# Gate logits of the fifth token group on VectorE within the last group of a fused attention and mixture-of-experts kernel, with a new order of the routing steps

## The chip, the cores and the metric

The kernel runs on one core of a Trainium2 chip. The metric is the device time of one execution in microseconds (us), taken as the median of several runs; lower is better.

## The reference

Three blocks follow one another. A linear attention with a decaying state gives a 3072 x 512 activation. A gated feed-forward block maps it through `(x @ w_a) * (x @ w_b) @ w_out` with 1536 hidden columns. A mixture of eight experts then sends each token to one expert.

```python
x = _moe_ref(x, ...)                        # (x @ w_a) * (x @ w_b) @ w_out
logits = x @ w_gate                         # 3072 x 8, the expert gates
e_idx = np.argmax(logits, axis=1)
probs = np.exp(logits - logits.max(-1, keepdims=True))
probs /= probs.sum(-1, keepdims=True) + 1e-09
gate_w = probs[np.arange(N), e_idx]
eom = 1.0 / (1.0 + np.exp(-(x @ w_output_gate)))   # 3072 x 8, the output gates
for e in range(E):
    mask = e_idx == e
    ye = np.maximum(x[mask] @ w1[e], 0.0) @ w2[e]
    out[mask] = gate_w[mask, None] * eom[mask, e, None] * ye
```

## The kernel before, in words

The 3072 tokens are cut into six groups of 512 (g = 0 to 5), each of four tiles of 128 tokens. In the feed-forward stage every group runs twelve steps, f = 0 to 11. In step f TensorE makes the two products of 128 hidden columns (`pe_up`, 24 matmuls of 512 columns, the b half first and then the a half) and after it the output product of the step before (`down`, 12 matmuls). VectorE multiplies the halves into `g_sb`, ScalarE rounds that to `g_hi`, VectorE makes the rest `g_lo`, and `down(f)` waits for `g_lo(f)`. Step 0 has no `down` of its own group ahead of it, but the last `down` of the group before has been issued already, so step 1 follows step 0 after 24 matmuls. After step 11 ScalarE evicts the group's output to `y_sb` and SyncE stores it to `x_rows` in the chip's memory.

The gates of group g - 1 are worked out during group g, from `y_sb`. The work has five parts: the 16 logits of each token, `dve_choose` (the best expert of each token), `dve_seen` (a running count of tokens by expert, which signals `seen_done`), the rank of each token within its expert (two small matmuls in `pe_rank`, which waits for `seen_done`, and `dve_rank`), and the scale (`dve_own_gate` picks the output gate of the chosen expert, `dve_scale` writes `t_scale`).

The logits of groups 0 to 3 are row products on VectorE (`dve_dots`): 64 instructions of 128 x 512, one for each of 16 gate columns and each of four tiles. Each reads a gate row that SyncE has broadcast to all partitions; there are four row buffers, so row e is loaded once the products of row e - 4 are done. `DOTS_AT` says how many of the 64 products stand in each step. The logits of group 4, which are worked out in the last group, g = 5, are made on TensorE: in steps 0 to 3 it transposes one tile each (`pe_yT`), in step 4 it multiplies by the gates (`pe_partial`) and in step 5 it adds the partial sums (`pe_logits`), and VectorE copies each result out of bank 3.

The first expert tiles (slots) are gathered ahead of time, from the tokens of groups 0 to 4 alone. `dve_off_hot` and `dve_first_hot` make one-hot tables from the ranks, `pe_first_slots` sorts with 20 small matmuls, and `dve_first_slots` writes the indices and signals `first_ready`. GpSimd's gathers 0 and 1 wait for `first_ready`, for the stored rows of group 4 (`x_out`) and for its stored scales (`scale_out`, which follows `t_scale` by one SyncE transfer). TensorE transposes the tile of gather 0 (`x_T`) after the `pe_up` of step 11 and ahead of `down(10)`. Every queue is in program order; nothing is scheduled at run time.

Of the kernel before, what the change touches and what calls it, by code (L numbers as in the profile page):

```python
# [5 lines left out]
F32R = mybir.dt.float32r  # L6
# [6 lines left out]
P = 128  # L13
# [15 lines left out]
GT = 512  # L29
# [63 lines left out]
def build(nc, steps_in, weights_in, gates_in, w1_in, w2_in, const_in, xT_dram, x_dram, out):  # L93
# [114 lines left out]
    gate_row = [place(f"gate_row{n}", (P, DM)) for n in range(GATE_SLOTS)]  # L208
    products_at = at[0]
    products = place("products", (P, DM))  # L210
    yT_sb = place("yT_sb", (P, KD, GT), where=yT_sb_at)
    part_sb = place("part_sb", (P, GT), where=products_at)
    gates_T = place("gates_T", (P, P), where=products_at)
    assert yT_sb_at + KD * GT * 4 <= products_at

    at[0] = products_at
    id_first = place("id_first", (P, TILES - TG))
    eq_first = place("eq_first", (P, TILES - TG, FIRST))
    hot_first = place("hot_first", (P, TILES - TG, FIRST), F32R)
    inv_first = place("inv_first", (P, FIRST))  # L220
    pad = place("pad", (P, 1))


    at[0] = common
# [44 lines left out]
    tl_i, tl_e, tl_run = (place(f"tl_{n}", (P, COLS + 1)) for n in range(3))  # L269
    tl_cmp, tl_cmp2 = (place(f"tl8_{n}", (P, COLS + 1, NE)) for n in range(2))  # L270
    off_hot = place("off_hot", (P, TILES, P), F32R)
    assert at[0] <= w2_lo_at + 2 * KE * DM * 4

    bank = [nc.alloc_psum_tensor(f"bank{i}", [P, 512], F32).ap() for i in range(8)]
# [363 lines left out]
    seen_done, rank_done, rank_read = sem("seen_done"), sem("rank_done"), sem("rank_read")  # L638


    AT_PART, AT_LOGITS = TG, TG + 1
    AT_CHOOSE, AT_GATE, AT_SCALE, AT_RANK = 6, 7, 8, 9
    DOT_CHOOSE, DOT_SEEN, DOT_RANK, DOT_SCALE = 6, 7, 10, 11
    LINKS = 15 + TG
    AT_FIRST = 10
    AT_W1_HI = {5: (0, 1), 6: (2, 3)}
    AT_W1_LO = {AT_SCALE: (0, 1), AT_RANK: (2,), AT_FIRST: (3,)}
    FIRST_COUNT, COUNT = 8, 64
    first_linked, first_hot_done, first_slots_done, first_ready = (sem("first_linked"), sem("first_hot_done"),
                                                                   sem("first_slots_done"), sem("first_ready"))  # L650
# [138 lines left out]
    def act_ff(act):  # L789
        def group(g, s, first, last):  # L790
            for f in range(KF):
                n = g * KF + f
                act.wait_ge(b_done, n + 1)
                act.wait_ge(down_done, n - 1 + 2)
                nc.scalar.copy(b_sb[:, f % 2], b_bank(f)).then_inc(b_read, 1)  # L795
                act.wait_ge(g_done, n + 1 + 2)
                nc.scalar.copy(g_hi[:, f % 2], g_sb[:, f % 2]).then_inc(g_hi_done, 1)  # L797
                if f == 3 and not first and not last:
                    split_x_hi(act, g + 1, 1 - s)
                if first and f + 2 < KF:  # L800
                    split_w_hi(act, f + 2)
                if last and f in AT_W1_HI:
                    split_w1(act, True, 0, AT_W1_HI[f])
                if not first:
                    if f == (AT_GATE if last else DOT_SEEN):
                        act_exp(act, g - 1)
                    if f == (AT_SCALE if last else DOT_SCALE):
                        act_exp_og(act, g - 1)
            if last:
                split_w2(act, True, 0, (0, 1, 2))  # L810
            act.wait_ge(down_done, KF * (g + 1) + 2)
            if not first:
                act.wait_ge(x_out, 16 * g)
                if not last:
                    act.wait_ge(dots_done, DOTS * g)
            for t in range(TG):
                nc.scalar.copy(y_sb[:, t, :], bank[4 + t]).then_inc(y_read, 1)

        in_groups(act, group)
# [8 lines left out]


    def on_pe(g):  # L830
        return g - (GROUPS - 2)

    def apart(g):
        return bank[7] if isinstance(g, int) and g == GROUPS - 1 else spare

    def pe_yT(pe, g, t):
        pe.wait_ge(y_read, TG * g + t + 1)
        if t == 0:
            pe.wait_ge(rank_read, g + 1)
        else:  # L840
            pe.wait_ge(yT_read, TG * on_pe(g) + t)
        for k in range(KD):
            ins = nc.tensor.transpose(spare[:, k * P:(k + 1) * P], y_sb[:, t, k * P:(k + 1) * P], ident)
        ins.then_inc(yT_done, 1)

    def pe_partial(pe, g, yT=yT_sb):

        pe.wait_ge(yT_read, TG * (on_pe(g) + 1))
        pe.sem_inc(waited, 1)
        for k in range(KD):  # L850
            strip = slice(k * (P // KD), (k + 1) * (P // KD))
            ins = nc.tensor.matmul(apart(g)[strip], gates_pad[:, k, :], yT[:, k, :], start=True, stop=True)  # L852
        ins.then_inc(part_done, 1)

    def pe_logits(pe, g, part=part_sb):
        pe.wait_ge(part_read, on_pe(g) + 1)
        for t in range(TG):
            ins = nc.tensor.matmul(apart(g)[:, t * 2 * NE:(t + 1) * 2 * NE], part[:, t * P:(t + 1) * P], sel, start=True, stop=True)
        ins.then_inc(logit_done, TG)

    def dve_yT(dve, g, t):
        dve.wait_ge(yT_done, TG * on_pe(g) + t + 1)
        nc.vector.tensor_copy(yT_sb[:, :, t * P:(t + 1) * P], spare.rearrange("p (k t) -> p k t", k=KD)).then_inc(yT_read, 1)

    def dve_partial(dve, g, part=part_sb):
        dve.wait_ge(part_done, on_pe(g) + 1)
        nc.vector.tensor_copy(part, apart(g)).then_inc(part_read, 1)

# [4 lines left out]
    def pe_rank(pe, g):  # L873

        pe.wait_ge(seen_done, g + 1)
        if on_pe(GROUPS - 2) <= (on_pe(g) if isinstance(g, int) else -1):
# [81 lines left out]
    def dve_off_hot(dve, t0, t1):  # L958

        nc.vector.tensor_tensor(off_hot[:, t0:t1], under(iota, t1 - t0), over(t_off[:, t0:t1], P), ALU.is_equal)  # L960
# [26 lines left out]
        if half == 1:  # L987
            ins.then_inc(first_slots_done, 1)

    ROUTE_STEPS = {AT_CHOOSE: dve_choose, AT_GATE: dve_gate, AT_SCALE: dve_scale, AT_RANK: dve_rank}  # L990
    def dve_rank_own(dve, g, link):
        dve_rank(dve, g, link)
        dve_own_gate(dve, g, link)

    DOT_STEPS = {DOT_CHOOSE: dve_choose, DOT_SEEN: dve_seen, DOT_RANK: dve_rank_own, DOT_SCALE: dve_scale}

    def dve_dots(dve, g, f):

        for n in range(sum(DOTS_AT[:f]), sum(DOTS_AT[:f + 1])):
            e, t = n // TG, n % TG  # L1000
            if e == 0:
                dve.wait_ge(y_read, TG * g + t + 1)
# [7 lines left out]
    def dve_ff(dve):  # L1010
        first_link = linker(dve, 0, first_linked)[0]

        def group(g, s, first, last):
            link = linker(dve, (g - 1) * LINKS) if not first else None
            for f in range(KF):
# [18 lines left out]
                        if f == DOT_SCALE:  # L1034
                            assert link[1][0] == LINKS, link[1]
                if last:
                    if f < TG:
                        dve_yT(dve, g - 1, f)
                    elif f == AT_PART:
                        dve_partial(dve, g - 1)  # L1040
                    elif f == AT_LOGITS:
                        dve_logits(dve, g - 1)
                    elif f in ROUTE_STEPS:
                        ROUTE_STEPS[f](dve, g - 1, link[0])
                        if f == AT_RANK:
                            assert link[1][0] == LINKS, link[1]
                if last:
                    known = TILES - TG
                    if AT_CHOOSE <= f <= AT_GATE:
                        half = (known - TG) // 2  # L1050
                        dve_off_hot(dve, (f - AT_CHOOSE) * half, (f - AT_CHOOSE + 1) * half)
# [30 lines left out]
    def pe_ff(pe):  # L1082
# [27 lines left out]
        def group(g, s, first, last):  # L1110
            for f in range(KF):
                pe_up(pe, g, s, f)
                if first and f == 0:
                    nc.tensor.transpose(spare[:, 0:P], gates_pad.rearrange("p k e -> p (k e)"), ident).then_inc(gates_T_done, 1)
                if last:
                    if f < TG:
                        pe_yT(pe, g - 1, f)
                    elif f == AT_PART:
                        pe_partial(pe, g - 1)
                    elif f == AT_LOGITS:  # L1120
                        pe_logits(pe, g - 1)
                if not first and f == (AT_SCALE if last else DOT_RANK - 1):
                    pe_rank(pe, g - 1)
                if last and f == AT_FIRST:
                    pe_first_slots(pe, 0)
# [463 lines left out]
```

## Time and profile before

| | us |
|---|---|
| median of 3 runs (lowest, highest) | 1026.68 (1026.66, 1026.78) |
| the profiled execution's own time | 1026.76 |
| its span, first to last instruction | 1024.9 |
| TensorE busy in the span | 1016.0 |
| VectorE busy in the span | 554.7 |
| mean granted TensorE clock | 1.000 of full speed |

The time of an execution is its span and some 1.9 us around it. Times inside the trace are counted from the span's start. The last group's `pe_up` of step 0 starts at 570.97 us, and the transpose of the first gathered tile at 670.57 us.

### The profile page before, as it was taken

How to read it: one execution, taken by the hardware profiler on the slowest of the kernel's cores; microseconds unless marked ns; L12 is line 12 of the kernel's file. 1: busy time of each engine (PE TensorE's matmuls, PEld its weight loads, DVE VectorE, ACT ScalarE, POOL GpSimd, SP SyncE). 2: the span in 40 equal slices, each digit the busy share in tenths (PEclk: the TensorE clock that was granted, in tenths of full speed). 3: DMA queues.
4: the chain of work that ended last, by engine and by line, in shares of the span. 5: the costliest groups of instructions: out<-in, count | busy, mean ns of one | idle time of the engine just before them, and what ended most of it. 6: DMA issues, size and time to landing. Idle time of an engine off the chain costs nothing.

```text
span 1024.9 us, 17443 instructions
## 1 busy us (share of the span) xinstructions
PE 1016.0 (99%) x5771; PEld 840.7 (82%) x5772; DVE 554.7 (54%) x1214; ACT 283.7 (28%) x491; POOL 120.6 (12%) x108
## 2 busy tenths in 40 slices
PE   9999999999999999999999999999999999999998
PEld 6888888888888888888888878888888888888886
DVE  4455332677477738773877223465644635354642
ACT  3544332121221122112211212141433423333431
POOL 5781000000000000000000000001111222211211
PEclk9999999999999999999999999999999999999999
DMA  9999400511151123104210212021753424254311
GB/s 360 378 336 317 114 1 0 154 52 42 30 135 49 34 57 115 56 21 108 68 52 21 83 42 83 1 62 56 274 198 124 146 101 165 84 174 158 117 39 37
DMA packets 53737, 113.93 MB, mean 111 GB/s; under 512 B 8741, under 2 KB 23525, under 8 KB 53168
## 3 DMA queue, kind: packets, MB, share of 16 engines
q1 hardware_dynamic: 48896, 99.21, 30.2%
q0 software_dynamic: 4480, 13.91, 4.0%
q8 instruction: 30, 0.49, 0.2%
q14 instruction: 27, 0.22, 0.1%
q10 hardware_dynamic: 304, 0.09, 0.0%
HBM read 96.37 MB, written 17.61 MB: 111 GB/s over the span
## 4 chain that ended last, share of the span: by engine, by line
PE 97%; DVE 1%; DMA 1%; issue 0%; ACTq 0%; POOL 0%; ACT 0%; DVEq 0%; POOLq 0%
PE bank L1078 38%; PE bank L1106 19%; PE bank L1439 15%; PE bank L1463 14%; PE bank L1447 2%; PE bank L564 2%; PE bank L594 2%; PE bank L671 1%; DVE probs L522 1%; PE bank L608 1%; PE bank L576 1%; DMA triu<-in_consts 1%; PE bank L1162 0%; PE bank L985 0%; PE bank L852 0%
## 5 line engine op out<-in xcount | busy, mean ns | idle before, releaser
L1078 PE MATMUL bank<-x_hi,wab_hi 128*128 128x512 f32 x576 | 224.4, 390 | 0.2 <-issue 0.2
L1078 PE MATMUL bank<-x_hi,wab_lo 128*128 128x512 f32 x576 | 224.2, 389 | 0.0
L1078 PE MATMUL bank<-x_lo,wab_hi 128*128 128x512 f32 x576 | 224.1, 389 | 0.0
L1007 DVE SCALAR_TENSOR_TENSOR products<-y_sb,gate_row 128x512 f32<-128x512 f32 x256 | 176.8, 691 | 22.5 <-DMA gate_row<-xT_dram 15.1
L1439 PE MATMUL bank<-w,xe 128*128 (+1 forms) x648 | 158.9, 399 | 0.5 <-DVE xe L695 0.5
L1019 DVE TENSOR_TENSOR g_sb<-bank,b_sb 128x512 f32<-128x512 f32 x72 | 49.7, 690 | 172.9 <-PE bank L1078 172.9
L1439 PEld LDWEIGHTS bank<-w,xe 128*128 128x128 f32 x648 | 119.3, 188 | 28.2 <-issue 1.8
L1078 PEld LDWEIGHTS bank<-x_hi,wab_hi 128*128 128x128 f32 x576 | 108.1, 188 | 22.9 <-issue 0.4
L1078 PEld LDWEIGHTS bank<-x_hi,wab_lo 128*128 128x128 f32 x576 | 108.1, 188 | 22.5
L1078 PEld LDWEIGHTS bank<-x_lo,wab_hi 128*128 128x128 f32 x576 | 108.2, 188 | 22.3
L1106 PE MATMUL bank<-wo_hi,g_hi 128*128 128x512 f32 x288 | 113.4, 394 | 0.0
L1106 PE MATMUL bank<-wo_hi,g_lo 128*128 128x512 f32 x288 | 112.2, 390 | 0.0
L1106 PE MATMUL bank<-wo_lo,g_hi 128*128 128x512 f32 x288 | 112.1, 389 | 0.0
L1379 POOL DMA_INDIRECT xg<-x_rows,idx_gather x28 | 35.3, 1259 | 633.7 <-DVE idx_gather L977 586.1
L797 ACT CAST g_hi<-g_sb 128x512 fp32r<-128x512 f32 x72 | 44.7, 621 | 230.4 <-DVE g_sb L1019 230.4
L795 ACT COPY b_sb<-bank 128x512 f32<-128x512 f32 x72 | 42.3, 587 | 213.4 <-PE bank L1078 213.3
L1463 PE MATMUL bank<-w_hi,hT_hi 128*128 (+1 forms) x208 | 83.7, 403 | 0.1
L1463 PE MATMUL bank<-w_hi,hT_lo 128*128 (+1 forms) x208 | 81.3, 391 | 0.0
L1463 PE MATMUL bank<-w_lo,hT_hi 128*128 (+1 forms) x208 | 81.1, 390 | 0.0
L1021 DVE TENSOR_TENSOR g_lo<-g_sb,g_hi 128x512 fp32r<-128x512 f32 x72 | 49.8, 692 | 49.5 <-ACT g_hi L797 49.5
L1171 DVE TENSOR_TENSOR hT_lo<-bank,hT_hi 128x512 fp32r<-128x512 f32 x52 | 33.5, 684 | 73.8 <-ACT hT_hi L1308 73.8
L1106 PEld LDWEIGHTS bank<-wo_hi,g_hi 128*128 128x128 f32 x288 | 54.1, 188 | 11.6 <-issue 0.8
(179 smaller groups left out, 1074.4 us busy)
## 6 DMA issues: line engine op xcount, KB each, us to landing
raw<-in_w SPq DMA_DIRECT2D x64, 512.0 KB, 5.6
gate_row<-xT_dram SPq DMA_DIRECT2D x64, 256.0 KB, 3.1
rows<-in_steps SPq DMA_DIRECT2D x20, 768.0 KB, 7.5
rows<-in_steps SPq DMA_DIRECT2D x24, 256.0 KB, 8.4
wab_raw<-in_weights SPq DMA_DIRECT2D x24, 256.0 KB, 9.4
x_rows<-y_sb SPq DMA_DIRECT2D x6, 1024.0 KB, 8.5
xT_dram<-x_all SPq DMA_DIRECT2D x4, 1024.0 KB, 13.9
x_raw<-xT_dram SPq DMA_DIRECT2D x16, 256.0 KB, 7.6
```

Of the source, the lines that this page charges most:

```text
L564: ins = nc.tensor.matmul(bank[2 * i + o][:, cols], kT[half_p, cols], qT[half_p, cols], start=True, stop=True)
L795: nc.scalar.copy(b_sb[:, f % 2], b_bank(f)).then_inc(b_read, 1)
L797: nc.scalar.copy(g_hi[:, f % 2], g_sb[:, f % 2]).then_inc(g_hi_done, 1)
L1007: nc.vector.scalar_tensor_tensor(products, y_sb[:, t], 1.0, gate_row[e % GATE_SLOTS], ALU.mult, ALU.mult, accum_out=L3[:, t, e:e + 1]).the ...
L1019: nc.vector.tensor_tensor(g_sb[:, f % 2], a_bank(f), b_sb[:, f % 2], ALU.mult).then_inc(g_done, 1)
L1021: nc.vector.tensor_tensor(g_lo[:, f % 2], g_sb[:, f % 2], g_hi[:, f % 2].bitcast(F32), ALU.subtract).then_inc(g_lo_done, 1)
L1078: ins = nc.tensor.matmul(to, wab(w, f, j), x[s][:, k, :], start=(k == 0 and m == 0), stop=(k == KD - 1 and m == 2))
L1106: ins = nc.tensor.matmul(bank[4 + t], gp[:, f % 2, toks], wo(w, f), start=(f == 0 and m == 0), stop=(f == KF - 1 and m == 2))
L1171: nc.vector.tensor_tensor(low[:, 4 * o:4 * o + 4].rearrange("p k t -> p (k t)"), bank[2 + o], high[:, 4 * o:4 * o + 4].rearrange("p k t -> ...
L1379: nc.gpsimd.indirect_dma_start(out=xg_first[s] if i < FIRST else xg[s], out_offset=None, in_=x_rows[0:rows_there], in_offset=bass.Indirect ...
L1439: ins = nc.tensor.matmul(bank[o], x[:, s, k, :], w[:, bass.ds(half + (k * FE + o * 512), 512)], start=(k == 0 and m == 0), stop=(k == KD - ...
L1463: ins = nc.tensor.matmul(bank[5 + s], h[:, k, :], w[:, bass.ds(half + k * DM, DM)], start=(k == 0 and m == 0), stop=(k == KE - 1 and m == 2))
```

## The change

The logits of group 4 are made by `dve_dots` too, within the last group. A second table, `LAST_DOTS_AT`, spreads the 64 products over steps 0 to 9. TensorE's 16 transposes and its two rounds of gate products for that group go, and VectorE's copies of them. The steps of the routing move: choose from step 6 to 4, seen from 7 to 5, `pe_rank` from 8 to 6 and `dve_rank` from 9 to 7, the first slots from 10 to 9, the own gate from 7 to 9 and the scale from 8 to 10. The splits of the first expert's weights stand in steps 10 and 11. SyncE loads 16 gate rows between the weights. The evicting of group 5's output on ScalarE now waits for the products in this group too. The tables of the first slots lie at another address, since the product buffer is used now.

```diff
--- before.py
+++ after.py
@@ -42,6 +42,7 @@
 DOTS_AT = (4, 7, 7, 3, 7, 6, 6, 6, 7, 7, 4, 0)
+LAST_DOTS_AT = (6, 8, 8, 8, 4, 6, 7, 5, 7, 5, 0, 0)
...
@@ -638,13 +636,13 @@
-    AT_PART, AT_LOGITS = TG, TG + 1
-    AT_CHOOSE, AT_GATE, AT_SCALE, AT_RANK = 6, 7, 8, 9
+    AT_CHOOSE, AT_SEEN, AT_RANK, AT_GATE, AT_SCALE = 4, 5, 7, 9, 10
     DOT_CHOOSE, DOT_SEEN, DOT_RANK, DOT_SCALE = 6, 7, 10, 11
     LINKS = 15 + TG
-    AT_FIRST = 10
+    AT_FIRST = AT_GATE
     AT_W1_HI = {5: (0, 1), 6: (2, 3)}
-    AT_W1_LO = {AT_SCALE: (0, 1), AT_RANK: (2,), AT_FIRST: (3,)}
+    AT_W1_LO = {10: (0, 1, 2), 11: (3,)}
+    AT_OFF_HOT = {0: (0, 2 * TG), AT_CHOOSE: (2 * TG, 4 * TG)}
...
@@ -762,12 +760,15 @@
+                load_gate_rows(sp, g, range(6))
                 for half in range(2):
                     sp.wait_ge(a_done, g * KF + 2 * half + 2)
                     load_expert(sp, raw1, w1_in, 0, raw1_in, (2 * half, 2 * half + 1))
+                    load_gate_rows(sp, g, range(3 * half + 6, 3 * half + 9))
                 for half in range(2):
                     sp.wait_ge(a_done, g * KF + 2 * half + 6)
                     load_expert(sp, raw2, w2_in, 0, raw2_in, (2 * half, 2 * half + 1))
+                    load_gate_rows(sp, g, range(3 * half + 12, min(3 * half + 15, 2 * NE)))
...
@@ -802,7 +803,7 @@
-                    if f == (AT_GATE if last else DOT_SEEN):
+                    if f == (AT_SEEN if last else DOT_SEEN):
                         act_exp(act, g - 1)
...
@@ -987,16 +973,16 @@
-    ROUTE_STEPS = {AT_CHOOSE: dve_choose, AT_GATE: dve_gate, AT_SCALE: dve_scale, AT_RANK: dve_rank}
...
+    LAST_STEPS = {AT_CHOOSE: dve_choose, AT_SEEN: dve_seen, AT_RANK: dve_rank, AT_GATE: dve_own_gate, AT_SCALE: dve_scale}
...
@@ -1034,21 +1020,14 @@
                 if last:
-                    if f < TG:
-                        dve_yT(dve, g - 1, f)
-                    elif f == AT_PART:
-                        dve_partial(dve, g - 1)
-                    elif f == AT_LOGITS:
-                        dve_logits(dve, g - 1)
...
+                    known = TILES - TG
+                    dve_dots(dve, g - 1, f, LAST_DOTS_AT)
+                    if f in LAST_STEPS:
+                        LAST_STEPS[f](dve, g - 1, link[0])
...
+                    if f in AT_OFF_HOT:
+                        dve_off_hot(dve, *AT_OFF_HOT[f])
...
@@ -1112,14 +1091,7 @@
-                if last:
-                    if f < TG:
-                        pe_yT(pe, g - 1, f)
-                    elif f == AT_PART:
-                        pe_partial(pe, g - 1)
-                    elif f == AT_LOGITS:
-                        pe_logits(pe, g - 1)
-                if not first and f == (AT_SCALE if last else DOT_RANK - 1):
+                if not first and f == (AT_RANK - 1 if last else DOT_RANK - 1):
                     pe_rank(pe, g - 1)
```

The first place is on VectorE, at `seen`, in the last group. A row is a source line, an operation, its output and inputs, and `x3` where it repeats. Before, in step 7:

```order
L1019 TENSOR_TENSOR g_sb<-bank,b_sb 128x512
L1021 TENSOR_TENSOR g_lo<-g_sb,g_hi 128x512
L923 TENSOR_TENSOR g_4_66<-g_3_65,L_61 128x32
L924 TENSOR_REDUCE g_3_71<-g_4_66 128x4
L928 COPY seen<-seen 128x8
L930 TENSOR_TENSOR seen<-seen,g_3_65 128x8 x3
L931 TENSOR_TENSOR seen<-seen,g_3_65 128x8
L960 TENSOR_TENSOR off_hot<-route_tab,t_off 128x1024
```

In the changed kernel, in step 5:

```order
L1005 TENSOR_TENSOR g_sb<-bank,b_sb 128x512
L1007 TENSOR_TENSOR g_lo<-g_sb,g_hi 128x512
L993 SCALAR_TENSOR_TENSOR products,L_61<-y_sb,gate_row_116 128x512 x2
L993 SCALAR_TENSOR_TENSOR products,L_61<-y_sb,gate_row_117 128x512 x4
L914 COPY seen<-seen 128x8
L916 TENSOR_TENSOR seen<-seen,g_3_65 128x8 x3
L917 TENSOR_TENSOR seen<-seen,g_3_65 128x8
L1005 TENSOR_TENSOR g_sb<-bank,b_sb 128x512
```

Six row products now stand between `g_lo` and the count `seen`, and the own gate (L923, L924) has left the step.

The second place is on VectorE at `t_scale`. Before, in step 8:

```order
L1019 TENSOR_TENSOR g_sb<-bank,b_sb 128x512
L1021 TENSOR_TENSOR g_lo<-g_sb,g_hi 128x512
L937 TENSOR_REDUCE g_2_70<-g_1_63 128x4
L938 TENSOR_SCALAR g_2_70<-g_2_70 128x4
L939 RECIPROCAL g_2_70<-g_2_70 128x4
L941 TENSOR_SCALAR g_4_72<-g_4_72 128x4
L942 RECIPROCAL g_4_72<-g_4_72 128x4
L943 TENSOR_TENSOR t_scale<-g_2_70,g_4_72 128x4
L711 TENSOR_TENSOR w_132<-raw_129,w_132 128x1024 x2
```

In the changed kernel, from the end of step 9 to the end of step 10:

```order
L962 TENSOR_SCALAR inv_first<-bank 128x2
L963 CAST idx_gather<-inv_first 128x2
L1005 TENSOR_TENSOR g_sb<-bank,b_sb 128x512
L1007 TENSOR_TENSOR g_lo<-g_sb,g_hi 128x512
L923 TENSOR_REDUCE g_2_70<-g_1_63 128x4
L924 TENSOR_SCALAR g_2_70<-g_2_70 128x4
L925 RECIPROCAL g_2_70<-g_2_70 128x4
L927 TENSOR_SCALAR g_4_72<-g_4_72 128x4
L928 RECIPROCAL g_4_72<-g_4_72 128x4
L929 TENSOR_TENSOR t_scale<-g_2_70,g_4_72 128x4
L709 TENSOR_TENSOR w_125<-raw_122,w_125 128x1024 x3
```

The scale stands two steps later, behind the first slots' indices instead of two steps ahead of them.

The third place is on SyncE, at the start of the last group, with the semaphores that each row waits for. Before:

```order
L774 DMA x_rows<-y_sb 128x4x512
L722 REGISTER_ALU
L722 COMPARE_AND_BRANCH
L729 DMA raw_129<-in_w 128x1024 [waits a_done]
L729 DMA raw_129<-in_w 128x1024
```

In the changed kernel:

```order
L775 DMA x_rows<-y_sb 128x4x512
L720 REGISTER_ALU
L720 COMPARE_AND_BRANCH
L749 DMA gate_row_116<-xT_dram 128x512
L749 DMA gate_row_117<-xT_dram 128x512
L749 DMA gate_row_118<-xT_dram 128x512
L749 DMA gate_row_119<-xT_dram 128x512
L749 DMA gate_row_116<-xT_dram 128x512 [waits dots_done]
L749 DMA gate_row_117<-xT_dram 128x512 [waits dots_done]
L727 DMA raw_122<-in_w 128x1024 [waits a_done]
L727 DMA raw_122<-in_w 128x1024
```

The loads of the gate rows come right behind the store of group 4's output, and ahead of the first weights.

## Rows read from the trace of the kernel before

**Rows 1.** Section 1 of the page: busy time of TensorE and others

```profile
PE 1016.0 (99%) x5771; PEld 840.7 (82%) x5772; DVE 554.7 (54%) x1214; ACT 283.7 (28%) x491; POOL 120.6 (12%) x108
```

**Rows 2.** Timeline of TensorE, last group: start, us, engine, line, operation

```profile
570.97 0.39 PE L1078 MATMUL bank<-x_hi,wab_hi 128*128 128x512 f32 x1
...
621.32 0.39 PE L1078 MATMUL bank<-x_hi,wab_hi 128*128 128x512 f32 x1
...
629.48 0.39 PE L1078 MATMUL bank<-x_hi,wab_hi 128*128 128x512 f32 x1
...
643.08 0.30 PE L879 MATMUL bank<-g,route_tab 128*128 128x32 f32 x2
...
670.57 0.60 PE L671 MATMUL bank<-ident,xg 128*128 128x128 f32 x4
```

**Rows 3.** Timeline of VectorE, steps 0 to 2 of group 4

```profile
484.32 0.69 DVE L1007 SCALAR_TENSOR_TENSOR products<-y_sb,gate_row 128x512 f32<-128x512 f32 x1 [4.05 <-DMA gate_row<-xT_dram]
...
485.05 0.69 DVE L1007 SCALAR_TENSOR_TENSOR products<-y_sb,gate_row 128x512 f32<-128x512 f32 x1
...
487.14 0.69 DVE L1019 TENSOR_TENSOR g_sb<-bank,b_sb 128x512 f32<-128x512 f32 x1
...
494.14 0.69 DVE L1019 TENSOR_TENSOR g_sb<-bank,b_sb 128x512 f32<-128x512 f32 x1
```

**Rows 4.** Line 1007, all its instructions: what they idled for (us, times)

```profile
  DMA gate_row<-xT_dram: 15.1, 4
```

**Rows 5.** Timeline of SyncE's queue

```profile
475.12 0.40 SPq L774 DMA_DIRECT2D x_rows<-y_sb  x1
...
573.56 0.40 SPq L774 DMA_DIRECT2D x_rows<-y_sb  x1
...
646.50 0.40 SPq L744 DMA_DIRECT2D x_rows<-t_scale  x1
```

**Rows 6.** Timeline of VectorE, last group

```profile
628.95 0.18 DVE L907 TENSOR_REDUCE g<-L 128x4 f32<-128x32 f32 x1
...
630.37 1.23 DVE L960 TENSOR_TENSOR off_hot<-route_tab,t_off 128x1024 fp32r<-128x1024 f32 x1
...
637.43 0.16 DVE L928 COPY seen<-seen 128x8 f32<-128x8 f32 x1
...
638.22 0.17 DVE L931 TENSOR_TENSOR seen<-seen,g 128x8 f32<-128x8 f32 x1
638.31 1.22 DVE L960 TENSOR_TENSOR off_hot<-route_tab,t_off 128x1024 fp32r<-128x1024 f32 x1
...
643.28 0.69 DVE L1019 TENSOR_TENSOR g_sb<-bank,b_sb 128x512 f32<-128x512 f32 x1 [3.75 <-PE bank L1078]
...
646.31 0.16 DVE L943 TENSOR_TENSOR t_scale<-g,g 128x4 f32<-128x4 f32 x1
...
664.60 0.17 DVE L977 CAST idx_gather<-inv_first 128x2 int32<-128x2 f32 x1
```

**Rows 7.** Tile t_scale: SyncE's stores of it, from issue to landing

```profile
DMA to landing us min/median/max: 2.4/2.8/3.3
```

**Rows 8.** Timeline of GpSimd, and line 1379 from 665 to 667

```profile
665.74 1.23 POOL L1379 DMA_INDIRECT xg<-x_rows,idx_gather  x1 [586.11 <-DVE idx_gather L977]
...
DMA to landing us min/median/max: 3.5/3.5/3.5
```

**Rows 9.** Line 774 from 573 to 575: the store of group 4's output

```profile
DMA to landing us min/median/max: 7.5/7.5/7.5
```

**Rows 10.** Timeline from 708.4 to 709.8: VectorE releases TensorE

```profile
708.50 0.42 DVE L695 TENSOR_TENSOR xe<-bank,xe 128x256 fp32r<-128x256 f32 x1
...
709.23 0.96 PE L1439 MATMUL bank<-w,xe 128*128 x3 [0.53 <-DVE xe L695]
```

**Rows 11.** Windows at the span's end: busy time by engine, clock, DMA

```profile
1020.00:1024.00 4.00, 0.01 (x1) 0.00 (x0) 0.75 (x1) 0.00 (x0) 1.00 (x1) 1.00 0.09 33
1024.00:1024.90 0.90, 0.00 (x0) 0.00 (x0) 0.00 (x0) 0.00 (x0) 0.00 (x0) 0.84 0.00 0
```

More of the change, by code:

```diff
@@ L210, in build @@
     products = place("products", (P, DM))
-    yT_sb = place("yT_sb", (P, KD, GT), where=yT_sb_at)
-    part_sb = place("part_sb", (P, GT), where=products_at)
     gates_T = place("gates_T", (P, P), where=products_at)
     assert yT_sb_at + KD * GT * 4 <= products_at
[L216 to L221, printed above, removed]
     at[0] = common
@@ L271, in build @@
     off_hot = place("off_hot", (P, TILES, P), F32R)
+    id_first = place("id_first", (P, TILES - TG))
+    eq_first = place("eq_first", (P, TILES - TG, FIRST))
+    hot_first = place("hot_first", (P, TILES - TG, FIRST), F32R)
+    inv_first = place("inv_first", (P, FIRST))
+    pad = place("pad", (P, 1))
     assert at[0] <= w2_lo_at + 2 * KE * DM * 4
@@ L813, in group @@
                 act.wait_ge(x_out, 16 * g)
-                if not last:
-                    act.wait_ge(dots_done, DOTS * g)
+                act.wait_ge(dots_done, DOTS * g)
             for t in range(TG):
@@ L830, in on_pe, with pe_partial @@
     def on_pe(g):
-        return g - (GROUPS - 2)
+        return g - (GROUPS - 1)
     def apart(g):
         return bank[7] if isinstance(g, int) and g == GROUPS - 1 else spare
[L836 to L846, printed above, removed]
+    def pe_partial(pe, g, yT):
         pe.wait_ge(yT_read, TG * (on_pe(g) + 1))
@@ L853, in pe_partial, with pe_logits @@
         ins.then_inc(part_done, 1)
-    def pe_logits(pe, g, part=part_sb):
+    def pe_logits(pe, g, part):
         pe.wait_ge(part_read, on_pe(g) + 1)
@@ L859, in pe_logits, with dve_partial @@
         ins.then_inc(logit_done, TG)
[L861 to L865, printed above, removed]
+    def dve_partial(dve, g, part):
         dve.wait_ge(part_done, on_pe(g) + 1)
@@ L875, in pe_rank @@
         pe.wait_ge(seen_done, g + 1)
-        if on_pe(GROUPS - 2) <= (on_pe(g) if isinstance(g, int) else -1):
+        if isinstance(g, int) and on_pe(g) >= 0:
             pe.wait_ge(logit_read, TG * (on_pe(g) + 1))
@@ L993, in dve_rank_own, with dve_dots @@
         dve_own_gate(dve, g, link)
+    LAST_STEPS = {AT_CHOOSE: dve_choose, AT_SEEN: dve_seen, AT_RANK: dve_rank, AT_GATE: dve_own_gate, AT_SCALE: dve_scale}
     DOT_STEPS = {DOT_CHOOSE: dve_choose, DOT_SEEN: dve_seen, DOT_RANK: dve_rank_own, DOT_SCALE: dve_scale}
-    def dve_dots(dve, g, f):
-        for n in range(sum(DOTS_AT[:f]), sum(DOTS_AT[:f + 1])):
+    def dve_dots(dve, g, f, dots_at=DOTS_AT):
+        for n in range(sum(dots_at[:f]), sum(dots_at[:f + 1])):
             e, t = n // TG, n % TG
@@ L1036, in group @@
                 if last:
-                    if f < TG:
-                        dve_yT(dve, g - 1, f)
-                    elif f == AT_PART:
-                        dve_partial(dve, g - 1)
-                    elif f == AT_LOGITS:
-                        dve_logits(dve, g - 1)
-                    elif f in ROUTE_STEPS:
-                        ROUTE_STEPS[f](dve, g - 1, link[0])
-                        if f == AT_RANK:
-                            assert link[1][0] == LINKS, link[1]
-                if last:
[L1048 to L1051, printed above, removed]
+                    known = TILES - TG
+                    dve_dots(dve, g - 1, f, LAST_DOTS_AT)
+                    if f in LAST_STEPS:
+                        LAST_STEPS[f](dve, g - 1, link[0])
+                        if f == AT_SCALE:
+                            assert link[1][0] == LINKS, link[1]
+                    if f in AT_OFF_HOT:
+                        dve_off_hot(dve, *AT_OFF_HOT[f])
                     if f == AT_RANK:
@@ L1114, in group @@
                     nc.tensor.transpose(spare[:, 0:P], gates_pad.rearrange("p k e -> p (k e)"), ident).then_inc(gates_T_done, 1)
-                if last:
-                    if f < TG:
-                        pe_yT(pe, g - 1, f)
-                    elif f == AT_PART:
-                        pe_partial(pe, g - 1)
-                    elif f == AT_LOGITS:
-                        pe_logits(pe, g - 1)
-                if not first and f == (AT_SCALE if last else DOT_RANK - 1):
+                if not first and f == (AT_RANK - 1 if last else DOT_RANK - 1):
                     pe_rank(pe, g - 1)
```

## The prediction

> **What bounds the kernel now.** I read the page's busy times first. TensorE is busy for 1016.0 of 1024.9 us [rows 1], so the end moves by what TensorE is spared, less what it is made to wait. Then the timeline of TensorE in the last group [rows 2], where the change acts, then VectorE, SyncE and GpSimd around it, to see what TensorE would wait for.
>
> A plain step of 36 matmuls takes 629.48 - 621.32 = 8.16 us [rows 2], so a `pe_up` alone (24 of them) takes 5.44 and a `down` 2.72. From the `pe_up` of step 0 at 570.97 to that of step 7 at 629.48 are 58.51 us. Seven `pe_up` and six `down` would be 7 x 5.44 + 6 x 2.72 = 54.40. The rest is the work that the change removes.
>
> **What is removed: 58.51 - 54.40 = 4.11 us of TensorE.** Four rounds of transposes, the gate products and the logits. Nothing else of TensorE goes; the rank matmuls and the first slots keep their price and only move. VectorE's copies go as well, from an engine that is not the bound.
>
> **What is added on VectorE, and when it can start.** A row product takes 485.05 - 484.32 = 0.73 us, and four of them 487.14 - 484.32 = 2.82 [rows 3], so n take 2.82 + 0.73 (n - 4). Step 1 of group 4, with seven, takes 494.14 - 487.14 = 7.00. Seven products are 5.01, so the opening (`g_sb`, the wait for `g_hi`, `g_lo`) is 1.99.
>
> The first product needs a gate row, and the rows are queued behind the store of `y_sb`. In group 4 the store is issued at 475.12 [rows 5] and the first product starts at 484.32, after an idle 4.05 [rows 3]: 9.20 later. Over four groups this idle time sums to 15.1, 3.78 each [rows 4], so I take 9.20 - 0.27 = 8.93. In the last group the store is issued at 573.56 [rows 5] in the same way: the first product starts at 582.5. The bounds: the store with nothing behind it lands in 7.5 [rows 9], which gives 581.1; group 4's own offset gives 582.8.
>
> From there VectorE's queue is full. Choose takes 630.37 - 628.95 = 1.42; `off_hot` of eight tiles 1.23, of which 0.08 lies inside its neighbour (the row at 638.22 lasts 0.17 and the next starts 0.09 later), so 1.15; seen 638.22 + 0.17 - 637.43 = 0.96 [rows 6].
>
> - Step 0: 6 products and 8 tiles of `off_hot`, 4.28 + 1.15: `g_sb(1)` starts at 587.9.
> - Steps 1 to 3: 8 products each, 7.00 + 0.73 = 7.73, three times: `g_sb(4)` at 611.1.
> - Step 4: 1.99 + 2.82 + 1.42 + 1.15 = 7.38: `g_sb(5)` at 618.5.
> - Step 5: 1.99 + 4.28 + 0.96 = 7.23: `seen_done` at 625.7.
>
> VectorE gains only 0.43 us on TensorE in an 8-product step, so the late start is carried along. In group 4 it doesn't matter: there seen is in step 7 and the rank matmuls follow in step 9.
>
> **First wait: the rank matmuls.** TensorE comes to them after the `pe_up` of step 6: 570.97 + 2 x 5.44 + 5 x 8.16 = 622.65. They follow `seen_done` by 709.23 - (708.50 + 0.42) = 0.31 [rows 10], so they start at 626.0. TensorE waits 3.39 us. Queued behind them are `down(5)` and all later steps, for which ScalarE and VectorE wait in turn. Some 0.3 of it is paid earlier: `g_lo(1)` ends at 587.9 + 1.99 + 0.08 = 590.0, and `down(1)` is due at 570.97 + 7 x 2.72 = 590.01. It isn't paid twice, since `seen_done` hangs on VectorE alone.
>
> **Second wait: the first gathered tile.** Before, from the rank matmuls (643.08) to the transposes of gather 0 (670.57) are 27.49 us, with all first-slot work in them [rows 2]. In the change two plain steps more lie between: 27.49 + 16.32 = 43.81, so TensorE reaches the transposes at 669.85, and the end of step 10's `pe_up`, one plain step earlier, is 661.69. By then VectorE has caught up. The scale is in step 10 now. The chain:
>
> - `g_sb(10)` 0.20 after that end (643.28 against 643.08, [rows 2, 6]): 661.89.
> - `t_scale` ends 646.31 + 0.16 - 643.28 = 3.19 later [rows 6], SyncE issues its store 0.03 later (646.50 after 646.47, [rows 5]): 665.11.
> - The store lands 2.8 later, 2.4 to 3.3 over six [rows 7]: 667.91.
> - GpSimd's gather starts 665.74 - 664.77 = 0.97 after its release [rows 6, 8]: 668.88. Waiting on the last of its three semaphores may save a part of that.
> - It lands 3.5 later [rows 8]: 672.38, and TensorE starts 0.31 later: 672.69.
>
> TensorE waits 672.69 - 669.85 = 2.84 us ahead of `down(10)`. Before, the gather landed at 669.24, 1.3 ahead of need, since `t_scale` was two steps earlier and only the indices were late.
>
> The Trainium skill ("DMA: Bandwidth & Descriptors", Anatomy of one DMA) puts a GpSimd DMA at 2.0 us plus its bytes over 436 GB/s. By that the gather (256 KB) would be 2.6 us, and a store of 2 KB 2.0, and the sum would come out 1.7 us lower. The rows of these very transfers (3.5 and 2.8) are higher, and I keep to them.
>
> Behind the transposes everything stands to TensorE as before. The gate rows 4 to 15 and the weights share SyncE's queue. The tightest place I find is row 6: it may load when 12 products are done (589.9 + 4.28 = 594.2), behind 1 MB of weights, and is wanted by product 25 (603.4 + 1.99 + 1.46 = 606.8). The first row, behind 1 MB of `y_sb`, took 8.9, which would be 603.1 here: hidden by VectorE's other products, so I cost it at nothing. Without that cover each us of it would lengthen the first wait by as much. ScalarE's new wait for the products at the end of the group is met in step 9.
>
> **The sum.** -4.11 + 3.39 + 2.84 = +2.12 us on the profiled 1026.76: 1028.88. That execution lies 0.08 above the median, so 1028.8. A gain of 4.11 is handed back twice over in waits.
>
> **The rivals.**
>
> *Both waits are absent* (faster). If the first row came at once, VectorE would start its products four us earlier and seen would be in time; and if gather 0 didn't need the scale, only 4.11 would count: 1022.6. Against it: four groups of four waited for the row [rows 4], and the gather's wait for the scale is in the code. It decides against me if the first product starts by 579.1 and `t_scale` reaches memory 2.8 earlier. Chance 0.07.
>
> *Only one wait.* The first alone: -4.11 + 3.39, 1026.0. The second alone: -4.11 + 2.84, 1025.4. For it speaks that the first falls by a full us for each us that the row lands earlier. Chance 0.12.
>
> *The clock falls* (slower still). TensorE now pauses for about 3 us twice. In the last stretch it did nothing from 1020.0 on; the granted clock was full until 1024.0 and 0.84 in the 0.9 us after that [rows 11]. So a pause of 4 us left it at its upper level, 2.4 GHz, once. If a pause did bring 1.2 GHz, one plain step at half speed would cost 8.2: 1037. The Trainium skill ("TensorE: Matmul & The Clock Gate", Why this matters for your kernels) warns of such gaps between bursts; by its rule this case would be likelier than I make it, by [rows 11] it is not. With any later wait that I have overlooked: chance 0.09.
>
> **How the numbers follow.** The two waits together hold 0.72. The row (1.4 down, 0.3 up), the store (0.4 down, 0.5 up), the gather's start (some 0.5 down) and small releases give this case a range of its own of 1027.4 to 1029.8. What a measurement of this kernel can tell from no change is 0.2%, 2.05 us, so the forecast of +2.1 lies on that bound: of the 0.72 I give 0.40 to slower and 0.32 to the same. With 0.12 of one wait the same has 0.44, slower has 0.40 + 0.09 = 0.49, and faster 0.07. Leaving out the fastest 0.07 and the clock, the range is 1025.4 to 1030.2.
>
> **What the profile after would show.** No transposes of `y_sb` in steps 0 to 3. An idle VectorE of some 4 us ahead of the first product in the last group, and 64 products of 0.69. TensorE idle some 3 us ahead of the rank matmuls, released by VectorE's `seen`, and some 3 us ahead of the transposes of gather 0, released by the gather. The prediction is wrong if either wait is missing, if a product waits for a later gate row, or if matmuls behind a pause run slower than 0.39.

## The result and the profile after

The changed kernel takes 1034.17 us (median of 4 executions, 1033.22 to 1035.52) against 1026.73 for the kernel before (4 executions beside them): a ratio of 1.0070, 95% interval 1.0058 to 1.0082. It is 7.4 us slower, 5.4 above the forecast of 1028.8 and above the range. The profiled execution took 1034.36 us with a span of 1032.6, against 1026.76 and 1024.9.

The page's busy times after, TensorE and VectorE. TensorE's busy time is nearly that of [rows 1], though 4.11 us of its work is gone: matmuls at half the clock, shown below, are busy for longer.

```profile
PE 1015.4 (98%) x5739; PEld 840.8 (81%) x5740; DVE 596.7 (58%) x1336; ACT 283.8 (27%) x491; POOL 120.7 (12%) x108
```

The view of waits, TensorE, after (engine and line, what released it, us in total, times, longest):

```profile
PE bank L865 <- DVE seen L917: 3.7, 1, 3.7
PE bank L669 <- DMA xg<-x_rows,idx_gather: 2.4, 1, 2.4
PE bank L612 <- DVE probs L535: 1.4, 1, 1.4
PE bank L562 <- DMA rows<-in_steps: 1.2, 1, 1.2
PE bank L1057 <- DVE wab_lo L350: 1.1, 1, 1.1
```

The first two are the two waits that were forecast. The two rows at the bottom lie in the attention stage and at its end, far ahead of the change; they vary between executions. All the feed-forward stage lies some 0.7 us later here, its last group 0.69. The timeline of TensorE after, at the two places (answers to [rows 2]; the duration is that of the pipelined matmul, so read the distance from start to start):

```profile
622.97 0.39 PE L1057 MATMUL bank<-x_lo,wab_hi 128*128 128x512 f32 x1
623.19 0.39 PE L1057 MATMUL bank<-x_hi,wab_lo 128*128 128x512 f32 x1
627.31 0.64 PE L865 MATMUL bank<-g,route_tab 128*128 128x32 f32 x2 [3.73 <-DVE seen L917]
...
628.76 0.63 PE L1085 MATMUL bank<-wo_lo,g_hi 128*128 128x512 f32 x1
629.19 0.63 PE L1085 MATMUL bank<-wo_hi,g_lo 128*128 128x512 f32 x1
...
633.43 0.40 PE L1057 MATMUL bank<-x_hi,wab_hi 128*128 128x512 f32 x1
633.66 0.40 PE L1057 MATMUL bank<-x_lo,wab_hi 128*128 128x512 f32 x1
...
673.84 0.39 PE L1057 MATMUL bank<-x_hi,wab_lo 128*128 128x512 f32 x1
676.67 0.66 PE L669 MATMUL bank<-ident,xg 128*128 128x128 f32 x4 [2.44 <-DMA xg<-x_rows,idx_gather]
...
677.39 0.39 PE L1085 MATMUL bank<-wo_lo,g_hi 128*128 128x512 f32 x1
...
678.34 0.63 PE L1085 MATMUL bank<-wo_lo,g_hi 128*128 128x512 f32 x1
678.77 0.63 PE L1085 MATMUL bank<-wo_hi,g_lo 128*128 128x512 f32 x1
...
681.49 0.39 PE L1085 MATMUL bank<-wo_hi,g_hi 128*128 128x512 f32 x1
...
684.22 0.60 PE L669 MATMUL bank<-ident,xg_first 128*128 128x128 f32 x4
```

Here stands what the prediction had at nothing. Behind each wait matmuls start 0.43 us apart (628.76, 629.19) instead of 0.23 (633.43, 633.66). The windows name the cause. After the times come busy us by engine; the number behind the last bracket is the granted clock, then DMA share and GB/s:

```profile
626.00:626.50 0.50, 0.00 (x0) 0.00 (x0) 0.47 (x4) 0.00 (x0) 0.00 (x0) 1.00 0.08 29
626.50:627.00 0.50, 0.00 (x0) 0.00 (x0) 0.43 (x3) 0.00 (x0) 0.00 (x0) 0.57 0.00 0
...
628.00:633.00 5.00, 5.00 (x13) 3.97 (x14) 4.21 (x12) 2.41 (x3) 0.00 (x0) 0.50 0.08 29
...
677.00:678.00 1.00, 1.00 (x7) 0.81 (x6) 1.00 (x3) 1.00 (x2) 0.00 (x0) 0.88 0.42 156
678.00:681.00 3.00, 3.00 (x9) 2.33 (x8) 2.97 (x4) 0.45 (x1) 0.00 (x0) 0.50 0.00 0
681.00:682.00 1.00, 1.00 (x6) 0.85 (x5) 0.12 (x1) 0.00 (x0) 0.00 (x0) 0.91 0.00 0
```

A granted clock of 0.50 is the lower level, 1.2 GHz. The first fall comes while TensorE stands still, the second only after the matmuls have begun again (full at 677.39, half at 678.34). SyncE's queue and VectorE after, with the start and end of the late chain (answers to [rows 3, 5, 6]):

```profile
574.25 0.40 SPq L775 DMA_DIRECT2D x_rows<-y_sb  x1
```

```profile
582.81 0.69 DVE L993 SCALAR_TENSOR_TENSOR products<-y_sb,gate_row 128x512 f32<-128x512 f32 x1 [3.44 <-DMA gate_row<-xT_dram]
...
583.62 0.69 DVE L993 SCALAR_TENSOR_TENSOR products<-y_sb,gate_row 128x512 f32<-128x512 f32 x1
...
588.52 0.68 DVE L1005 TENSOR_TENSOR g_sb<-bank,b_sb 128x512 f32<-128x512 f32 x1
...
627.09 0.17 DVE L917 TENSOR_TENSOR seen<-seen,g 128x8 f32<-128x8 f32 x1
...
669.15 0.16 DVE L929 TENSOR_TENSOR t_scale<-g,g 128x4 f32<-128x4 f32 x1
```

And the chain that ended last, between `t_scale` and the gathered tile (start, us, what):

```profile
669.34 2.64 DMA x_rows<-t_scale
...
673.01 3.61 DMA xg<-x_rows,idx_gather
```

**Where the 7.7 us of span come from.** (1) The later start: 574.25 - 573.56 = +0.69. (2) The removed work: -4.11. (3) First wait: without it TensorE would come to the rank matmuls at 622.65 + 0.68 = 623.33 (the forecast's time and the shift of step 0, whose matmuls begin 0.68 later); it comes at 627.31: +3.98. (4) The clock behind it: from there to the next `pe_up` are 633.43 - 627.31 = 6.12 us; the same work at full clock takes 649.71 - 646.40 = 3.31 (in the run with eleven added products, below): +2.81. (5) Second wait: from 673.84 + 0.23 = 674.07 to 676.67, +2.60. (6) The clock behind it: 684.22 - 676.67 = 7.55, against 673.53 - 667.60 = 5.93 in the last run below: +1.62. The sum is +7.59, with 0.1 left over. Term (4) is that of this one execution; the profiles of experiment 3 show a smaller one behind the same wait. Waits and clock had to be told apart by experiments, since one trace can't show that the slow matmuls would be gone with the pause.

### The profile page after: what moved, and what is told of

It is laid out like the page before. It is cut to its first block, busy times and chain, and to the rows that moved or that the text cites. A ratio compares the mean times of both kernels' runs of the same rounds, so it can differ in the third digit from the quotient of the medians.

```text
span 1032.6 us, 17529 instructions
## 1 busy us (share of the span) xinstructions
PE 1015.4 (98%) x5739; PEld 840.8 (81%) x5740; DVE 596.7 (58%) x1336; ACT 283.8 (27%) x491; POOL 120.7 (12%) x108
## 4 chain that ended last, share of the span: by engine, by line
PE 89%; DVE 5%; DMA 3%; issue 1%; ACT 1%; SPq 0%; POOL 0%; DVEq 0%; POOLq 0%; ACTq 0%
PE bank L1057 34%; PE bank L1085 18%; PE bank L1411 15%; PE bank L1435 14%; DVE products L993 2%; PE bank L1419 2%; DMA rows<-in_steps 2%; PE bank L562 1%; PE bank L592 1%; PE bank L669 1%; DMA gate_row<-xT_dram 1%; PE bank L606 1%; DVE probs L520 1%; PE bank L574 1%; DVE g_lo L1007 0%
## 5 line engine op out<-in xcount | busy, mean ns | idle before, releaser
L993 DVE SCALAR_TENSOR_TENSOR products<-y_sb,gate_row 128x512 f32<-128x512 f32 x320 | 221.1, 691 | 29.7 <-DMA gate_row<-xT_dram 19.1
L1085 PEld LDWEIGHTS bank<-wo_hi,g_lo 128*128 128x128 f32 x288 | 55.1, 191 | 11.7
```

The source lines that it names most:

```text
L993: nc.vector.scalar_tensor_tensor(products, y_sb[:, t], 1.0, gate_row[e % GATE_SLOTS], ALU.mult, ALU.mult, accum_out=L3[:, t, e:e + 1]).the ...
L1085: ins = nc.tensor.matmul(bank[4 + t], gp[:, f % 2, toks], wo(w, f), start=(f == 0 and m == 0), stop=(f == KF - 1 and m == 2))
```

## The experiments

The main theory: two waits of 4.0 and 2.6 us, and 4.4 us for half-rate matmuls that the pauses bring on. A rival: the waits alone, with the slow matmuls due to something else in this stretch (transfers, VectorE's products), so that they stay when the pauses go. Kernels of a group ran beside the same executions of the kernel before, whose median was 1027.42 (29 executions) for `fill_rank`, `fill_both`, `rows_early` and `xT_late`, 1027.41 (17) for `both`, `pause8` and `pause11`, and 1026.96 (14) for `scale9` and `best`. "Over before" is the difference to that. Each profile is of one execution of its kernel.

**1. The pauses filled.** `fill_rank` puts 14 matmuls of 512 columns, whose result isn't used, ahead of the rank matmuls; `fill_both` also puts nine ahead of the first gathered tile. No data are brought forward, only TensorE doesn't stand still for as long.

```diff
@@ pe_ffn, last group, fill_rank @@
+                if last and f == AT_RANK - 1:
+                    for _ in range(14):
+                        nc.tensor.matmul(spare, x_hi[s][:, 0, 0:P], x_hi[s][:, 0, :], start=True, stop=True)
@@ fill_both, these too @@
                 if last and f == KF - 1:
+                    pe.wait_ge(first_ready, 1)
+                    for _ in range(9):
+                        nc.tensor.matmul(spare, x_hi[s][:, 0, 0:P], x_hi[s][:, 0, :], start=True, stop=True)
```

> The changed kernel with 14 more matmuls of 512 columns into bank 3 ahead of the rank matmuls, 14 x 0.227 = 3.2 us of work in a wait of 3.7 us. Clock theory: the pause is what brings 1.2 GHz, so with the engine busy the rank matmuls start at the same time, behind VectorE, but they and the 12 matmuls of the output product run at the full rate; 2.9 us less than the changed kernel, 1031.2. Rival, the slow matmuls have another cause (transfers or VectorE beside them): no change, 1034.2. Second rival, seen_done isn't what is waited for: the added matmuls lengthen the time by 3.2, 1037.4.

> As fill_rank, and 9 more such matmuls (2.0 us) ahead of the transposes of the first gathered tile, where 2.6 us are waited. Clock theory: neither pause costs clock, 2.9 + 1.6 = 4.5 us less than the changed kernel, 1029.6; that is also what the prediction's waits alone would give with this start. Rival, another cause: 1034.2. Rival, only a pause of over 3 us counts: the second fill brings nothing beyond fill_rank, 1031.2.

Measured: `fill_rank` 1030.71 us (8 executions), ratio 1.0033 (1.0023 to 1.0044), 3.3 over before. `fill_both` 1029.70 (10), ratio 1.0021 (1.0011 to 1.0030), 2.3 over before. The profile of `fill_rank`, one row of waits and one of windows:

```profile
PE bank L865 <- DVE seen L917: 0.5, 1, 0.5
...
625.00:630.00 5.00, 4.48 (x23) 3.45 (x22) 4.11 (x14) 2.52 (x3) 0.00 (x0) 1.00 0.16 56
```

With the same late `seen_done` and a pause of 0.5 us left, the clock stays at 1.00. The two fills together took the changed kernel from 7.4 over before to 2.3 over it, 5.1 us, with nothing done to bring `seen` or the gather forward. The theory had 4.4, the rival nothing; the 0.7 between lies within what executions of one kernel differ by. So the slow matmuls are the pauses' doing.

**2. The first gate rows earlier.** Four buffers are free when the `y_sb` store is issued, so SyncE can load the first four rows ahead of that store, in every group.

```diff
@@ sync_ffn @@
-                load_gate_rows(sp, g, range(GATE_SLOTS))
...
-                load_gate_rows(sp, g, range(6))
+                load_gate_rows(sp, g, range(GATE_SLOTS, 6))
...
+            if not last:
+                load_gate_rows(sp, g + 1, range(GATE_SLOTS))
             sp.wait_ge(y_read, TG * (g + 1))
```

> The changed kernel with the first four gate rows of a group loaded ahead of the store of the last group's output, not behind it. Row theory: the first product starts right behind g_lo of step 0, 3.4 us earlier, the wait at the rank matmuls falls to about 0.3 us and no clock is lost there: 3.4 + 2.9 less, 1027.8. Rival, the wait at the rank matmuls comes from VectorE's load in steps 1 to 5 and not from the start: 1034.2, or with the start moved and the wait only shortened to 2 us, 1031.

Measured: 1028.19 us (10 executions), ratio 1.0007 (0.9998 to 1.0017), 0.8 over before. The wait for `seen` shrank to 0.2; the second stayed:

```profile
PE bank L669 <- DMA xg<-x_rows,idx_gather: 2.7, 1, 2.7
```

From 7.4 to 0.8 is 6.6 us, where the terms (3) and (4) make 6.79. Without the row queued behind the store the first wait is all but gone, and that wait with its clock is most of the loss.

**3. The gathered tile wanted later, or ready earlier.** `xT_late` puts the transposes behind `down(10)`. `scale9` works out the own gate and the scale both in step 9, so that the scale is stored some 6.7 us earlier; the wait on `seen_done` stays in both.

```diff
@@ xT_late @@
-                if last and f == KF - 1:
-                    x_T(pe, 0, 0, 0, spare)
                 if f > 0:
                     down(g, f - 1, first, (lambda: pe_first_slots(pe, 1)) if last and f == AT_FIRST else None)
+                if last and f == KF - 1:
+                    x_T(pe, 0, 0, 0, spare)
@@ scale9 @@
-    AT_CHOOSE, AT_SEEN, AT_RANK, AT_GATE, AT_SCALE = 4, 5, 7, 9, 10
+    AT_CHOOSE, AT_SEEN, AT_RANK, AT_GATE, AT_SCALE = 4, 5, 7, 9, 9
...
+    def dve_gate_scale(dve, g, link):
+        dve_own_gate(dve, g, link)
+        dve_scale(dve, g, link)
...
-    LAST_STEPS = {AT_CHOOSE: dve_choose, AT_SEEN: dve_seen, AT_RANK: dve_rank, AT_GATE: dve_own_gate, AT_SCALE: dve_scale}
+    LAST_STEPS = {AT_CHOOSE: dve_choose, AT_SEEN: dve_seen, AT_RANK: dve_rank, AT_GATE: dve_gate_scale}
```

> The changed kernel with the transposes of the first gathered tile issued behind the output product of step 10, 2.7 us later, not ahead of it. Gather theory: the gather lands just as TensorE gets there, so the wait of 2.6 us and the 1.6 us of clock behind it go: 1034.2 - 4.2 = 1030.0. Rival, the wait only moves to the next user of the tile (split of xe, then the first expert product): no gain, 1034.

> The changed kernel, with both the gate and the scale of the last group in step 9, so that t_scale is stored and the rows gathered about 6.7 us earlier; the wait on seen_done and everything else as in the changed kernel. Theory (the changed kernel pays 2.60 us for the wait of x_T on the gather and 1.64 us for the half-rate matmuls behind it): both go, 1034.2 - 4.2 = about 1030.0 us, with no wait of over 0.5 us left at L669 for the gathered rows and one of about 3.7 us left at L865. Rival (the gather is held by something else than t_scale): the wait on the gathered rows stays near 2.4 us and the time near 1034.

Measured: `xT_late` 1029.51 us (10 executions), ratio 1.0022 (1.0013 to 1.0032), 2.1 over before. `scale9` 1030.74 (7), ratio 1.0032 (1.0020 to 1.0044), 3.8 over before. In `scale9` the first wait is left as it was, and from 660 us on nothing is waited for and the clock is full:

```profile
PE bank L865 <- DVE seen L917: 3.7, 1, 3.7
...
660.00:690.00 30.00, 30.00 (x151) 1.00 0.22 53
```

Between 3.6 and 5.3 us came back, where terms (5) and (6) make 4.22. With the scale stored earlier the wait is gone: it was `t_scale` that held the gather, as the forecast had it.

These two profiles also show that term (4) isn't one number. Both keep the first wait of 3.7 us, but from the rank matmuls to the next `pe_up` are 631.47 - 626.57 = 4.90 us in `xT_late` and 632.31 - 627.42 = 4.89 in `scale9`, 1.6 over the 3.31 of full clock and not 2.81. In `xT_late` the clock fell only after the matmuls had begun again, and was back while they ran:

```profile
626.00:627.00 1.00, 0.43 (x4) 0.43 (x4) 0.93 (x4) 0.00 (x0) 0.00 (x0) 1.00 0.18 68
627.00:628.00 1.00, 1.00 (x5) 0.85 (x5) 0.31 (x2) 0.84 (x2) 0.00 (x0) 0.74 0.48 168
628.00:630.00 2.00, 2.00 (x6) 1.52 (x5) 1.93 (x6) 1.67 (x2) 0.00 (x0) 0.50 0.04 13
630.00:631.00 1.00, 1.00 (x3) 0.77 (x3) 0.97 (x3) 0.00 (x0) 0.00 (x0) 0.55 0.00 0
```

**4. Both waits treated.** `both` has the edits of `rows_early` and `xT_late`.

> The changed kernel with both edits, gate rows ahead of the store and the transposes of the first gathered tile behind the output product of step 10. If the two pauses and the clock behind them are all that the change costs, what is left is the 4.11 us of TensorE work removed: 1026.7 - 4.1 = 1022.6, or 1023 with what remains of the first wait. Rival, a wait stays or a new one opens behind (the split of the first tile, the weights): 1026 or more.

Measured: 1024.62 us (5 executions, 1022.78 to 1025.08), ratio 0.9964 (0.9950 to 0.9978), 2.8 under before. That is 1.6 short of the expected 1023, though two of the five, with 1022.78 and 1023.42, came near it. In the profile, which is of the slowest (1025.08), 0.8 us of the second wait is back, and the chain shows a longer transfer: the store of `t_scale` took 3.75 us instead of the 2.64 of the changed kernel, and the 2.72 us of `down(10)` didn't cover it.

```profile
PE bank L669 <- DMA xg<-x_rows,idx_gather: 0.8, 1, 0.8
...
662.58 3.75 DMA x_rows<-t_scale
```

**5. A pause put into the kernel before.** VectorE makes 8 or 11 products, whose result isn't used, one after the other ahead of `dve_seen` of the last group. No row, store or gather of the change is there.

```diff
@@ dve, before the change, pause8 (pause11: range(11)) @@
+    pause_done = sem("pause_done")
...
         dve_own_gate(dve, g, link)
+        if isinstance(g, int) and g == GROUPS - 2:
+            for n in range(8):
+                if n > 0:
+                    dve.wait_ge(pause_done, n)
+                nc.vector.tensor_tensor(yT_sb[:, 0, :], y_sb[:, 0, :], y_sb[:, 1, :], ALU.mult).then_inc(pause_done, 1)
         dve_seen(dve, g, link)
```

> The kernel before, with 8 products of 0.73 us added on VectorE ahead of seen in step 7 of the last group, so that its rank matmuls wait about 1.5 us. Clock theory: a short pause costs its own length and no clock, +1.5 us. Rival, any pause brings 1.2 GHz: +1.5 + 2.9 = +4.4.

> The kernel before, with 11 such products, so that its rank matmuls wait about 3.7 us, as those of the changed kernel do. Clock theory: the pause alone brings 1.2 GHz, with none of the change in place: +3.7 + 2.9 = +6.6 us. Rival, the clock fell for another reason in the change (row products, gate row loads): +3.7 only.

Measured: `pause8` 1028.68 us (10 executions), ratio 1.0014 (1.0005 to 1.0023), 1.3 over before, with a wait of 0.9 and a mean granted clock of 0.999 or 1.000 in all ten. `pause11` 1031.83 (6), ratio 1.0042 (1.0029 to 1.0054), 4.4 over before: between the two figures expected, and, as the mean clocks suggest, a median over two kinds of execution. Two took 1029.23 and 1030.10 with a mean clock of 1.000; four took 1031.57, 1032.09, 1032.49 and 1033.69 with one of 0.997 or 0.998. The profiled one is 1030.10: a pause of 3.07 us, and the clock holds.

```profile
642.95 0.39 PE L1084 MATMUL bank<-x_hi,wab_lo 128*128 128x512 f32 x1
646.40 0.41 PE L880 MATMUL bank<-g,route_tab 128*128 128x32 f32 x2 [3.07 <-DVE seen L937]
...
649.71 0.39 PE L1084 MATMUL bank<-x_hi,wab_hi 128*128 128x512 f32 x1
```

So a lower clock comes with a pause alone, without any of the change's transfers, but not in every execution. The four took 2.6 us more (median 1032.29 against 1029.67), near the 2.81 of term (4). The one profile is of an execution without the fall; that the clock of the four fell behind this pause is concluded from `pause8`, which has the same edit with a shorter pause and no mean clock under 0.999.

**6. The version that keeps the gain.** `best` has the edits of `rows_early` and `scale9`.

> The changed kernel with the first four gate rows of a group loaded ahead of the y store, and gate and scale of the last group both in step 9. Theory (the removed TensorE work of 4.11 us comes back in full once neither wait nor a fallen clock stands against it): 4.11 less about 0.2 us, so about 1023.3 us beside a kernel before of 1027.4, with no wait of over 0.5 us at L865 and L669. Rival (the moved gather meets other transfers, or another wait takes the place of the one on the gathered rows): 1024.6 us or more, as the run with the late x_T gave.

Measured: 1023.57 us (6 executions, 1023.34 to 1023.86), ratio 0.9963 (0.9950 to 0.9976), 3.4 under before and 10.6 under the changed kernel. TensorE waits 0.27 us ahead of the rank matmuls and not at all for the gathered tile; the stretch is at full clock:

```profile
623.69 0.41 PE L866 MATMUL bank<-g,route_tab 128*128 128x32 f32 x2 [0.27 <-DVE seen L918]
...
667.37 0.39 PE L1062 MATMUL bank<-x_hi,wab_lo 128*128 128x512 f32 x1
667.60 0.60 PE L669 MATMUL bank<-ident,xg 128*128 128x128 f32 x4
...
673.53 0.60 PE L669 MATMUL bank<-ident,xg_first 128*128 128x128 f32 x4
```

## Why the prediction was wrong

**The step that failed** is in the rival "The clock falls": "a pause of 4 us left it at its upper level, 2.4 GHz, once". From that I took matmuls behind a pause to start at their full rate, and gave the clock, with later waits, 0.09. Behind both pauses they ran at half rate, for 2.81 + 1.62 = 4.43 us together; the sum had no term for it. With the late start of the profiled execution (0.69) and the waits' own misses (+0.59 and -0.24, below) that makes the 5.5 us between its 1034.36 and the forecast's 1028.88. `fill_both` removes the falls with the waits' causes left alone and lands 2.3 us over before, where the sum had said +2.12: the rest of the sum was right, in part because the two misses lean opposite ways. The forecast's own sign of being wrong came up, matmuls behind a pause that last longer than 0.39 (0.63).

Why the rows misled: [rows 11] show one pause in one execution, and its second row, 0.84 in the last 0.9 us, can be read as the clock falling from 1.00 to 0.50 on the way. No matmul followed to show it. A row that can't show the dear case was set as evidence against it. The rival's price was wrong the other way: "8.2: 1037" took one plain step at half speed, for a total 8.2 above the sum; measured are 4.43 for the two falls, and 1.6 instead of 2.81 for the first in two other profiles.

The Trainium skill ("TensorE: Matmul & The Clock Gate", Why this matters for your kernels) advises against idle gaps of some microseconds between bursts of matmuls. The runs agree with it, for a pause of 3.7 us in each of 21 executions, read by the mean clock.

**Removed work, 4.11 us: right.** No transposes of `y_sb` are left in steps 0 to 3. `best` gives back 3.4 of it with 0.27 us of wait left; the 0.4 between is no more than what executions of the kernel before differ by.

**First wait, 3.39 us: right in place and cause, 0.59 short.** The first product starts 582.81 - 574.25 = 8.56 after the store (I had 8.93), `g_sb(1)` 14.27 (I had 587.9 - 573.56 = 14.34), and `seen_done` 627.26 - 0.69 = 626.57 instead of 625.73. That is 0.07 early at `g_sb(1)` and 0.84 late at `seen_done`, so the rest came up in steps 1 to 5. Seven products that start on a fresh row begin 0.80 or 0.81 after the one before, where I had taken 0.73 for all: 0.5 in sum. In group 4 of the kernel before, where I had it from, fresh rows show 0.73 too. The other 0.42 is one product in step 3:

```profile
606.99 0.69 DVE L993 SCALAR_TENSOR_TENSOR products<-y_sb,gate_row 128x512 f32<-128x512 f32 x1
...
608.14 0.69 DVE L993 SCALAR_TENSOR_TENSOR products<-y_sb,gate_row 128x512 f32<-128x512 f32 x1 [0.46 <-DVE products L993]
```

It is the first product of row 6, but the row isn't what it waits for: its load was issued at 594.97 and landed 4.7 later. All eight profiles with row products in the last group have this gap, always 0.46. What it is stays open. TensorE then started 627.31 - 627.26 = 0.05 after `seen_done`, not 0.31, which takes 0.26 off again.

**Second wait, 2.84 us: right, 0.24 too long.** The store of `t_scale` took 2.64 (2.8), the gather started 673.01 - 671.98 = 1.03 after it (0.97) and landed in 3.61 (3.5); TensorE followed within 0.1, sooner than the 0.31 I took.

**Costed at nothing, and right:** the later gate rows. VectorE idled 19.1 us for gate rows in five groups, against 15.1 in four [rows 4], and 3.44 of the difference is the first product's of the last group. Row 6, the tightest, was there at 599.7 (I had 603.1) and first wanted at 607.7.

**The rival "only one wait"** was priced at 1026.0 and 1025.4. `xT_late`, with the first wait alone, gave 1029.51, `rows_early`, with the second alone, 1028.19: 3.5 and 2.8 us higher. Some 0.7 of each is the kernel before, which took 1027.42 beside them; the rest, 2.8 and 2.1, is about the clock's share.

## What to carry to other kernels

When a change adds a pause of some microseconds to an otherwise full TensorE (here the clock fell behind pauses of 2.5 us and more, and not behind 0.9; nothing between was run), add to the pause what the matmuls behind it lose at half rate, unless a trace of the same program shows matmuls at full rate behind pauses of that length, in several executions. A small transfer that a busy engine needs soon should be queued ahead of a large store, and a result that starts a chain of store and gather should be worked out as early as its inputs allow: these two reorderings turned 7.4 us slower into 3.4 us faster. And an item costed at nothing on the strength of one row deserves the question whether that row could have shown the cost at all.

## What was not expected of the hardware

Whether a pause costs the clock is partly chance. Read by the mean granted clock of each execution (0.998 or less for a fall), with the pause's length from the one profiled execution: with a longest pause in the last group of 0.9 us (`pause8`) none of ten fell; with one of 2.5 us (`fill_rank`) five of eight and of 2.7 us (`rows_early`) eight of ten; of 3.1 us (`pause11`) four of six; of 3.7 us (the changed kernel, `xT_late`, `scale9`) all 21. One execution of `fill_rank`, counted among the five, shows 0.948 at 1031.55 us, which its time doesn't bear out; it stays unexplained. The reading is coarse: two of the 60 executions of the kernel before beside these runs show 0.998 too, and one of the ten of `fill_both` 0.997, and within `rows_early` the fastest execution, 1026.59 us, is among the eight. The traces of `fill_rank` and `rows_early` do show the fall itself, to 0.50 behind the wait for the gathered tile, and that of `fill_both` shows none.

How long the clock stays down isn't fixed either. It came back while matmuls ran on: in the changed kernel behind the first wait after 6.1 us of them, having fallen before they began, and behind the second some 3.4 us after it had fallen; in `xT_late` behind the first wait some 3.4 us after (an estimate from the windows above: 0.74 of 627 to 628 puts the fall at 627.5, 0.55 of 630 to 631 the return at 630.9). The same wait thus cost 2.8 us in one profile and 1.6 in two. What decides it in one execution, these runs don't show.
